# Retention output turned by its own matmuls, the mean of the layer norm spread by a matmul, and the inverse deviation moved behind the second MLP layer

## What is computed

```python
# retention: q, k, v are (2, 8, 768, 64)
for t in range(S):
    state = gamma * state + outer(k[:, :, t], v[:, :, t])
    y[:, :, t] = scale * q[:, :, t] @ state
x = y.transpose(0, 2, 1, 3).reshape(2, 768, 512)
# layer norm and MLP: 512 -> 2048 -> 512
mu = mean(x); var = mean((x - mu) ** 2)
xn = (x - mu) / sqrt(var + 1e-06) * g_ln
x = x + maximum(xn @ w_ch1, 0) @ w_ch2
# then the mixture of four causal attention experts, x (2, 768, 512) -> (2, 768, 512)
```

## Time and profile before

| what | value |
|---|---|
| median of 3 executions | 479.29 us (479.22 to 479.84) |
| the profiled execution | 479.44 us, its span 477.7 us, mean granted TensorE clock 0.998 |
| PE busy | 465.1 us (97%), 2850 matmul records |
| DVE busy | 257.0 us (54%), 595 instructions |
| ACT busy | 148.2 us (31%) |
| POOL busy | 133.1 us (28%) |
| DMA | 33.06 MB moved |

### The profile page before, as it was taken

One profiled execution on the slowest core, in us unless ns is written; L12 is line 12 of the kernel. 1 busy time (PEld: TensorE's weight loads), 2 busy tenths in 40 slices (PEclk: granted clock), 3 DMA queues, 4 the chain that ended last, 5 costly groups with the idle time before them and its releaser, 6 DMA issues.

```text
span 477.7 us, 7612 instructions
## 1 busy us (share of the span) xinstructions
PE 465.1 (97%) x2850; PEld 404.1 (85%) x2850; DVE 257.0 (54%) x595; ACT 148.2 (31%) x338; POOL 133.1 (28%) x165
## 2 busy tenths in 40 slices
PE   7999999999999999999999999999999899999896
PEld 6899988888888888888888888888999799998775
DVE  4657763222556536524673441142637889888833
ACT  2323323111111311111121111131425777777833
POOL 1000009999920000000002000000501567666710
PEclk9999999999999999999999999999999999999999
DMA  7968403444400000000013000000145444443024
GB/s 170 259 150 191 125 1 97 138 130 134 123 0 1 0 0 0 0 0 0 0 33 78 1 0 1 0 1 0 23 100 123 117 116 109 101 103 76 1 105 161
DMA packets 65793, 33.06 MB, mean 69 GB/s; under 512 B 47584, under 2 KB 61920, under 8 KB 65760
## 3 DMA queue, kind: packets, MB, share of 16 engines
q1 hardware_dynamic: 64960, 32.43, 26.6%
q10 hardware_dynamic: 800, 0.20, 0.2%
HBM read 20.03 MB, written 3.15 MB: 49 GB/s over the span
## 4 chain that ended last, share of the span: by engine, by line
PE 88%; DVE 6%; ACT 2%; issue 2%; POOL 1%; DMA 0%; POOLq 0%; ACTq 0%; DVEq 0%
PE ps L708 27%; PE ps L717 27%; PE ps L784 5%; PE ps L631 5%; PE ps L835 4%; PE ps L756 3%; PE ps L803 3%; PE ps L605 3%; PE ps L818 2%; PE ps L592 2%; PE ps L862 2%; DVE a L1448 2%; PE ps L622 2%; PE ps L645 1%; DVE a_low_lo L1456 1%
## 5 line engine op out<-in xcount | busy, mean ns | idle before, releaser
L1302 DVE SCALAR_TENSOR_TENSOR h_t_lo<-ps,h_t_hi 128x512 fp32r<-128x512 f32 x48 | 33.2, 692 | 146.5 <-ACT h_t_hi L992 146.5
L992 ACT ACTIVATE h_t_hi<-ps 128x512 fp32r<-128x512 f32 x48 | 28.7, 598 | 218.3 <-PE ps L708 218.3
L708 PE MATMUL ps<-xn_t_hi,w_hi 128*128 128x512 f32 x192 | 74.8, 389 | 0.0
L708 PE MATMUL ps<-xn_t_hi,w_lo 128*128 128x512 f32 x192 | 74.7, 389 | 0.0
L708 PE MATMUL ps<-xn_t_lo,w_hi 128*128 128x512 f32 x192 | 74.7, 389 | 0.0
L717 PE MATMUL ps<-w_hi,h_t_hi 128*128 128x512 f32 x192 | 74.7, 389 | 0.0
L717 PE MATMUL ps<-w_lo,h_t_hi 128*128 128x512 f32 x192 | 74.7, 389 | 0.0
L717 PE MATMUL ps<-w_hi,h_t_lo 128*128 128x512 f32 x192 | 74.7, 389 | 0.0
L550 POOL TENSOR_SCALAR a<-a,inv_den,weight 128x768 f32<-128x768 f32 (+5 forms) x48 | 34.1, 720 | 50.5 <-DVE inv_den L1468 50.1
L717 PEld LDWEIGHTS ps<-w_hi,h_t_hi 128*128 128x128 f32 x192 | 36.0, 188 | 7.5
L717 PEld LDWEIGHTS ps<-w_lo,h_t_hi 128*128 128x128 f32 x192 | 36.1, 188 | 7.5
(11 more groups left out here) (143 smaller groups left out, 879.0 us busy)
## 6 DMA issues: line engine op xcount, KB each, us to landing
raw_w<-in_moe_w_ch SPq DMA_DIRECT2D x32, 256.0 KB, 3.0
k_twice_hi<-pj_hi SPq DMA_DIRECT2D x32, 96.0 KB, 2.1
k_twice_lo<-pj_lo SPq DMA_DIRECT2D x32, 96.0 KB, 2.2
out_y<-out_sb SPq DMA_DIRECT2D x12, 256.0 KB, 2.0
raw_k<-in_k SPq DMA_DIRECT2D x7, 384.0 KB, 4.6
raw_q<-in_q SPq DMA_DIRECT2D x7, 384.0 KB, 5.1
raw_v<-in_v SPq DMA_DIRECT2D x7, 384.0 KB, 3.4
q_both<-pj_hi SPq DMA_DIRECT2D x16, 96.0 KB, 2.0
```

The source lines that it names most:

```text
L708: mm = pe.matmul(ps[:, f % 2, :], w1[a_][:, f, kk, :], xn_t[b_][:, kk, :], start=(kk == 0 and p_ == 0), stop=(kk == KT - 1 and p_ == 2))
L992: act.activation(h_t["hi"][:, f % 2, :], ps[:, f % 2, :], ACT.Relu).then_inc(s_hhi, 1)
L1302: dve.scalar_tensor_tensor(h_t["lo"][:, f % 2, :], ps[:, f % 2, :], 0.0, f32(h_t["hi"][:, f % 2, :]), ALU.max, ALU.subtract).then_inc(s_hl ...
```

## The change

- **Retention output turned.** In `chunk_outputs`, `raw["v"]` becomes the stationary operand (64 columns) and `prob` the moving one (128 columns), so the result has head dimensions as rows and positions as columns. The two heads of a pair go to the two halves of the PSUM partitions. In `state_outputs` the state is stationary and `q_t` moves. The two heads' states are laid as two blocks of a 128x128 matrix with zeros elsewhere, so one matmul serves both heads: 40 matmuls in place of 80. `chunk_outputs` now stands ahead of `state_outputs`.
- **States.** DVE writes each state in two halves (partitions 0 to 63 and columns 0 to 63, then 64 to 127 and 64 to 127): 2 copies and 8 additions a pair, where there were 1 and 4. POOL clears `state` and fills `mean_of` with 1/512 at the start.
- **Mean by matmul.** `x` now holds the turned output. DVE adds the four pairs of heads of a batch (`first_sum`; `add_heads` later), PE multiplies the sum by `mean_of`, which gives the mean on every partition (`first_mean` twice for block 0, 256 columns each; `next_mean` in blocks 0 and 1, 512 columns), DVE subtracts it (`centred`), and the split into high and low parts reads `centred`.
- **Inverse deviation behind the second layer.** Since relu(a*z) = a*relu(z) for a > 0, the factor `rstd` is applied to the block's result: the residual step becomes `rows = ps * rstd + rows`. `rows` is `x` turned back by DVE (`turn_rows`, 16 squares in slices f = 5 to 7 of the same block). Moments, root and Newton step move to slices 8 to 11 of the same block. Block 2, which had none of it, now has it too.
- **Removed:** `turn_first` (16 PE transposes), `turn_xn` (16 DVE transposes for each of blocks 1 and 2), the whole norm of block 0 ahead of the MLP. `turn_x2` takes slices 2 to 4 in place of 2 to 7.
- POOL's weight splitting now waits for the last `first_sum` in place of `xn`.

The diff, cut to its core:

```diff
             def chunk_outputs(it, g):
                 wait_loaded(pe, it, "v", g)
                 pe.wait_ge(s_prob, 2 * it + g + 1)
+                if it >= 1:
+                    pe.wait_ge(s_yx, y_turn(it - 1, g) + 1)
                 for c in range(G):
                     for j in range(2):
-                        mm = pe.matmul(y_bank(it, g, j)[:, c], prob[:, g, j, c, :], raw["v"][:, it % RB, j, G * g + c],
-                                       start=False, stop=True, skip_group_check=True)
+                        rows_ = slice(j * D, (j + 1) * D)
+                        pe.matmul(y_bank(g)[rows_, c * P:(c + 1) * P], raw["v"][:, it % RB, j, G * g + c], prob[:, g, j, c, :],
+                                  start=(c == 0), stop=(g == 0 and c == 0), skip_group_check=True)
+            def state_outputs(it, g):
+                pe.wait_ge(s_st, 2 * (NC - 1) * (it + 1))
+                for c in range(max(1, G * g), G * g + G):
+                    mm = pe.matmul(y_bank(g)[:, (c - G * g) * P:(c - G * g + 1) * P], state[:, it % 2, c - 1, :],
+                                   q_t[:, it % 2, c, :], start=False, stop=True, skip_group_check=True)
                 mm.then_inc(s_y, 1)
+            def first_mean(b):
+                pe.wait_ge(s_const, 6)
+                pe.wait_ge(s_acc, (HP - 1) * (b + 1))
+                pe.matmul(half_of(mean_bank(), b), mean_of[:, :], half_of(head_sum, b), start=True, stop=True,
+                          skip_group_check=True).then_inc(s_mean, 1)
...
-            key_values(0)
             for it in range(NIT - 1):
                 scores_of(it, 1)
-                state_outputs(it, 0)
+                if it == 0:
+                    key_values(0)
                 chunk_outputs(it, 0)
                 if it == NIT - 2:
                     key_values(it + 1)
+                state_outputs(it, 0)
                 for unit in range(0 if it == 0 else 2, 4):
                     turn(it + 1, unit)
                 scores_of(it + 1, 0)
+                chunk_outputs(it, 1)
                 if it < NIT - 2:
+                    key_values(it + 1)
                     state_outputs(it, 1)
-                    chunk_outputs(it, 1)
-                    key_values(it + 1)
                     for unit in (0, 1):
                         turn(it + 2, unit)
+                if it == HP:
+                    first_mean(0)
...
             def mlp(i, last):
                 for f in range(2, NF):
                     hidden(i, f)
                     project(i, f - 1)
+                    if not last and f == 12:
+                        next_mean(i)
...
# DVE
                 for c in range(1, NC - 1):
-                    dve.wait_ge(s_st, (NC - 1) * it + c)
-                    dve.tensor_tensor(state[:, it % 2, c], kv_bank()[:, c], state[:, it % 2, c - 1],
-                                      ALU.add).then_inc(s_st, 1)
+                    for j in range(2):
+                        half = slice(j * D, (j + 1) * D)
+                        dve.wait_ge(s_st, 2 * (NC - 1) * it + 2 * c + j - 1)
+                        dve.tensor_tensor(state[half, it % 2, c, half], kv_bank()[half, c], state[half, it % 2, c - 1, half],
+                                          ALU.add).then_inc(s_st, 1)
...
+                b, kk = divmod(it - 1, HP)
+                if it >= 2 and kk > 0:
+                    first_sum(b, kk)
+                if it == HP + 1:
+                    for kk in range(KT):
+                        first_centre(0, kk)
+                if it == HP + 2:
+                    for kk in range(KT):
+                        first_lo(0, kk)
                 apply_causal(it + 1, 0)
...
                 for tau in range(NT):
                     dve.wait_ge(s_o, NT * i + tau + 1)
-                    dve.tensor_tensor(xn_tile(tau), ps[:, 2 + tau, :].rearrange("p (k d) -> p k d", k=KT),
-                                      tile_of(i, tau), ALU.add).then_inc(s_x2, 1)
+                    dve.scalar_tensor_tensor(rows_tile(tau), ps[:, 2 + tau, :].rearrange("p (k d) -> p k d", k=KT),
+                                             rstd[:, tau:tau + 1], rows_tile(tau), ALU.mult, ALU.add).then_inc(s_x2, 1)
```

More of the change, by code:

```diff
@@ L118, in retention_moe_program @@
         g_col = sb(ctx, "g_col", [P, KT])
-        with ExitStack() as early:
-            state = sb(early, "state", [P, 2, NC - 1, D])
         with ExitStack() as late:
@@ L607, in scores_of @@
                 mm.then_inc(s_s, 1)
-            def state_outputs(it, g):
-                pe.wait_ge(s_st, (NC - 1) * (it + 1))
-                if y_first(it, g) == 0:
-                    pe.wait_ge(s_turned, 4 * NIT)
-                elif (it, g) == (NIT - 1, 1):
-                    pe.wait_ge(s_yx, y_turn(NIT - 1, 0) + 1)
-                elif y_turn(it, g) >= 1:
-                    pe.wait_ge(s_yx, y_turn(it, g))
-                first = max(1, G * g)
-                for c in range(first, G * g + G):
-                    for j in range(2):
-                        rows = slice(j * D, (j + 1) * D)
-                        pe.matmul(y_bank(it, g, j)[:, c - G * g], q_t[rows, it % 2, c, :], state[rows, it % 2, c - 1, :],
-                                  start=(c == first), stop=False, skip_group_check=True)
             def chunk_outputs(it, g):
@@ L720, in project, with next_mean @@
                         mm.then_inc(s_o, 1)
+            def next_mean(i):
+                pe.wait_ge(s_acc, (KT - 1) * i + sums_before(2))
+                pe.matmul(mean_bank(), mean_of[:, :], head_sum[:, :], start=True, stop=True).then_inc(s_mean, 1)
             def mlp(i, last):
@@ L1003, in mlp @@
                     hidden_hi(i, f)
-                    if f == 7 and not last:
-                        root(i + 1, 0)
+                    if f == 10:
+                        root(i)
                     if last and f == 12:
@@ L1284, in turn_xn, with moments, inverse @@
-            def turn_xn(n, q_):
+                chain = Chain(dve, s_ln, NORM_STEPS * n)
+                def moments():
+                    dve.wait_ge(s_rows, NQ * (n + 1))
+                    for tau in range(NT):
+                        chain.counted(dve.bn_stats(stats[:, tau, 0, :], rows_tile(tau)))
+                    chain.wait()
+                    for tau in range(NT):
+                        chain.counted(dve.bn_aggr(mean_var[:, tau, :], stats[:, tau, 0, :]))
+                def inverse():
+                    chain.wait()
+                    chain.then(dve.tensor_scalar(veps[:, :], mean_var[:, :, 1], LN_EPS, None, ALU.add))
+                    dve.reciprocal(rvar[:, :], veps[:, :]).then_inc(s_rvar, 1)
@@ L1342, in mlp @@
                     hidden_lo(i + 1, 1)
-            norm = normalise(0)[0]
-            moments, inverse, refine = (norm[n] for n in (slice(0, U), U, slice(U + 2, None)))
             for it in range(NIT - 1):
```

298 lines of the change are left out of this document (130 added, 168 removed).

## The result

The changed kernel takes 483.13 us (median of 4 executions, 482.30 to 483.65) against 479.37 for the kernel before beside it: 1.0075 times the time before, interval 1.0058 to 1.0093. It is slower by 0.75%. The forecast was 474.5, faster by 1%, with a range that ended at 479.0. The profiled execution took 483.22 us, its span is 481.5 us.

A forecast was written before the change was run, and what follows sets the result against it. PE bound the kernel before; after the change a loop of waits through DVE would decide the pairs. 1.15 - 6.15 + 0.2 - 1.5 + 1.5 = -4.8 us from 479.44, median 474.5 us, range 467.5 to 479.0.

The forecast's parts named there:

- the wait in the passage: PE ahead of chunk_outputs(7,0), released by DVE's mask: an idle time of 3.5 us, the new stall of this change.
- the start: Up to scores(1,0), with scores(0,1) ahead of the key values: scores(1,0) at about 16.6, 1.15 us more.
- the loop: Retention's pairs: a circle of waits through DVE takes 6.67 us a pair instead of 7.90, 6.15 us less over five.
- What bounds PE: Retention's steady part: PE is busy for all of a pair's 7.90 us; its sum falls by 1.30 to 6.60.
- the chunk outputs: PE in a retention pair: 0.77 us each, instead of 1.48 and 1.39, with two heads on separate array halves.
- the state outputs: PE in a retention pair: half as many whole-array instructions, 0.74 us for group 1 and 0.49 for group 0.
- The rival of unpaired heads: The two heads' chunk outputs don't run side by side: 1.54 us, PE's pair 8.14, total 484; chance 0.10.
- States: DVE in a retention pair: ten half-state instructions at 0.234 us each, 2.34 us instead of 1.17 for five.
- The rival of overlapping halves: DVE overlaps half states, 0.14 us each, 1.4 a pair; PE's 6.60 decides, total 471.3; chance 0.23.
- The passage: From scores(6,0) to the first `hidden`: 17.9 us instead of 19.39, 1.5 less, with PE's 3.5 us wait inside.
- the clock's fall: Behind the 3.5 us stall, 4.3 us of PE work takes twice that at the lower clock: 478.8; chance 0.10.
- The means: MLP blocks 0 and 1: one `next_mean` of 512 columns each on PE, 0.74 us apiece, 1.5 us more.

## Why half states are dear

Two copies of the kernel before, in which nothing but the five state instructions is cut in two: by partitions as in the change, or by columns. Count, elements and waits are the same in both. No chunk or state output is turned here. The first new instruction below is the cut by partitions (`half` is 64 partitions), the second the cut by columns (`half` is 32 columns); each copy has one of them.

```diff
                 for c in range(1, NC - 1):
-                    dve.wait_ge(s_st, (NC - 1) * it + c)
-                    dve.tensor_tensor(state[:, it % 2, c], ...)
+                    for j in range(2):
+                        dve.wait_ge(s_st, 2 * (NC - 1) * it + 2 * c + j - 1)
+                        dve.tensor_tensor(state[half, it % 2, c], ...)
+                        dve.tensor_tensor(state[:, it % 2, c, half], ...)
```

> The kernel before, with one edit: each state instruction is cut in two by partitions (0 to 63, 64 to 127; 64 columns each), ten a pair in place of five, and each waits only for the one before last, as in the changed kernel. PE's order is as before, so a pair has 2.6 us of idle DVE to take it. The changed kernel's ten took 2.54 us a pair where a wait for the one before last would have let two overlap. Theory: an instruction on the other half of the partitions does not begin until the one ahead has ended, so ten take 2.3 to 2.6 us a pair, against 1.17 now. Rival (it was the zero-padded 128-column layout or the busy PSUM that was slow): ten take 1.4 to 1.7. The pair stays 7.9 us by both, since the states are not on PE's path by more than 0.7 us; total within 1 us of before.

> The kernel before, with one edit: each state instruction is cut in two by columns (0 to 31, 32 to 63, all 128 partitions), ten a pair, each waiting for the one before last: the same count, the same elements and the same waits as the cut by partitions. Theory (the hold comes from the change of partitions): here neighbours overlap, ten take 1.3 to 1.7 us a pair. Rival (each small instruction costs its 0.23 to 0.25 whatever it touches): 2.3 to 2.6 us, as by partitions. Total within 1 us of before by both.

The timeline of DVE, by partitions first, then by columns:

```profile
62.85 0.48 DVE L1168 COPY state<-ps 64x64 f32<-64x64 f32 x2 [1.33 <-PE ps L645]
63.36 2.00 DVE L1173 TENSOR_TENSOR state<-ps,state 64x64 f32<-64x64 f32 x8
65.39 0.56 DVE L288 TENSOR_TENSOR scaled_k<-raw_k,decay_sb 128x384 f32<-128x384 f32 x1
```

```profile
50.80 0.29 DVE L1168 COPY state<-ps 128x32 f32<-128x32 f32 x2 [1.34 <-PE ps L645]
51.03 0.97 DVE L1173 TENSOR_TENSOR state<-ps,state 128x32 f32<-128x32 f32 x8
51.91 0.56 DVE L288 TENSOR_TENSOR scaled_k<-raw_k,decay_sb 128x384 f32<-128x384 f32 x1
```

From the copy to the scaling, ten take 65.39 - 62.85 = 2.54 us by partitions and 51.91 - 50.80 = 1.11 us by columns, 0.25 and 0.11 each. The half with 64 columns is longer than that with 32 by 32 x 1.04 ns = 0.03 us, which leaves 0.11 of the 0.14. So the price is in the change of partitions from one instruction to the next, not in the number of instructions. Nor is an addition on half the partitions slow in itself: its record lasts 0.222 us, that of a whole one 0.224. By columns, ten cost no more than the five whole ones of the earlier trace rows (1.17). The Trainium skill, VectorE: DVE Perf Modes, section "Two Vector instructions with no wait between them", states such a hold for an instruction that starts in another quadrant of partitions than the one before. The two traces agree with it, 0.25 us against 0.11. The theory holds, and "small instructions cost a fixed price" falls.

On the total I was wrong by partitions: 497.05 us (one execution), not within 1 us. The states of the kernel before are on PE's path after all: its state outputs wait for them, as they do not in the earlier trace rows.

```profile
56.31 0.66 PE L622 MATMUL ps<-state,q_t 64*128 64x64 f32 x8 [0.93 <-DVE state L1173]
```

The scores start at 49.93 and 59.04, so a pair takes 9.11 in place of 7.90 even where the clock is at 1.00, and the table of stretches shows it far below that in others:

```profile
16.00:24.00 8.00, 7.97 (x79) 6.76 (x79) 2.80 (x8) 3.22 (x8) 0.00 (x0) 0.75 0.82 186
40.00:48.00 8.00, 8.00 (x66) 7.25 (x64) 3.46 (x13) 1.47 (x3) 0.00 (x0) 0.54 0.52 118
```

By columns the time is 479.32 us (one execution), that of before (479.49).

## Start and passage: one edit each

Three versions of the changed kernel with its half states. First, `key_values(0)` stands ahead of `scores_of(0, 1)` again:

```diff
+            key_values(0)
             for it in range(NIT - 1):
                 scores_of(it, 1)
-                if it == 0:
-                    key_values(0)
```

> Changed kernel, but key_values(0) stands ahead of scores_of(0,1) again, as before the change. Theory 1: states(0) begin 0.9 us earlier, so scores(1,0) comes about 0.9 us earlier, 482.2 us. If the start's loss is the lower clock that follows PE's waits of 2.0 and 0.7 us there, the shorter waits may keep the clock up, and then it is 2 to 2.5 us earlier: 480.7 us.

Measured: 481.23 us median of 10 (479.20 to 483.30), 1.0033 of before (1.0013 to 1.0052). In the profiled execution scores(1,0) start at 16.47, 1.48 sooner: 0.94 because the key values run at 9.42 and not at 10.36, as the theory has it, the rest because the clock stayed up. But the wait in the passage is there as before, and this time the clock did not fall behind it (table of stretches, and PE's timeline):

```profile
64.00:66.00 2.00, 0.83 (x13) 0.69 (x13) 1.36 (x3) 0.00 (x0) 0.00 (x0) 1.00 0.00 0
66.00:68.00 2.00, 2.00 (x24) 1.88 (x22) 0.43 (x1) 0.98 (x2) 0.24 (x1) 1.00 0.03 8
```

```profile
65.17 0.88 PE L622 MATMUL ps<-prob,raw_v 128*64 128x128 f32 x12 [2.96 <-issue]
65.97 1.38 PE L631 MATMUL ps<-q_t,state 128*128 128x128 f32 x10
```

Same wait, 2.96 against 2.97 us; chunk outputs 0.88 against 1.55. The ten executions go with their mean granted clock: 479.2 and 479.5 us at 0.999; 480.4 to 481.0 at 0.995; 481.5 to 483.3 at 0.988 to 0.992. So behind two waits of one length the clock fell in one profile and not in the other, and one kernel differs from itself by 4 us.

Second, the splits of batch 0 move behind the mask of (7,0):

```diff
-                if it == HP + 2:
-                    for kk in range(KT):
-                        first_lo(0, kk)
                 apply_causal(it + 1, 0)
+                if it == HP + 2:
+                    for kk in range(KT):
+                        first_lo(0, kk)
```

> Changed kernel, but DVE's four splits of batch 0 (first_lo) stand behind the mask of (7,0) in place of ahead of it. Theory 1 (PE's wait of 3.0 us ahead of chunk_outputs(7,0) is DVE's queue): the wait falls by 1.65 us to 1.3 and the total by 1.6 us if the clock falls all the same, and by about 3.2 us (to 480) if the shorter wait keeps the clock at full. Rival (the wait has another cause, such as the states of pair 7): no change.

Measured: 480.11 us (479.00 to 480.77), 1.0008 (0.9998 to 1.0017), no difference from before. The wait is 1.37 in place of 2.97 and the clock is at 1.00 behind it, both as expected; the fall at the start is still there (0.50 at 18 to 20 us).

```profile
66.09 0.88 PE L622 MATMUL ps<-prob,raw_v 128*64 128x128 f32 x12 [1.37 <-issue]
66.89 1.38 PE L631 MATMUL ps<-q_t,state 128*128 128x128 f32 x10
```

Third, PE is kept busy in that wait with 22 transposes of the identity:

```diff
+            pe.wait_ge(s_turned, 4 * NIT)
+            for _ in range(22):
+                pe.transpose(ps[:, 0, 0:P], ident[:, :], ident[:, :])
             chunk_outputs(NIT - 1, 0)
```

> Changed kernel, and PE turns the identity 22 times into a free bank in its 3.0 us wait ahead of chunk_outputs(7,0); nothing else changes. If the granted clock of 0.50 behind that wait costs what the rows say (chunk outputs of 1.55 in place of 0.81 us, state outputs of 2.15 in place of 1.4), the clock stays at full and the total falls by 1.4 to 1.6 us, to 481.6. If the clock does not matter there because DVE ends last in the passage, no change.

Measured: 482.17 us (481.96 to 482.47), 1.0053 (1.0036 to 1.0069). Behind the fillers the ten state outputs take 1.38 in place of 2.23, yet the time is only 1.0 lower. Passage and MLP together gained 1.9 us between the profiles; the start lost 0.8 (0.4 of it lies ahead of scores(0,1) already, the rest is a fall of the clock that lasted longer than in the changed kernel), the last stage 0.3. The last run therefore fills all of PE's long waits: sixteen transposes ahead of the first state outputs, four ahead of the next turn, and the 22.

```diff
+                if it == 0:
+                    for _ in range(16):
+                        pe.transpose(ps[:, 7, 0:P], ident[:, :], ident[:, :])
                 state_outputs(it, 0)
                 for unit in range(0 if it == 0 else 2, 4):
+                    if it == 0:
+                        for _ in range((4, 0, 0, 0)[unit]):
+                            pe.transpose(ps[:, 7, 0:P], ident[:, :], ident[:, :])
                     turn(it + 1, unit)
```

> The changed kernel as it is, with idle transposes of the identity in PE's waits and nothing else: sixteen ahead of the first state outputs and four ahead of the first turn that follows, and 22 in the wait ahead of chunk_outputs(7,0) (these alone gave 482.17, with the clock falling at the start). Theory: without either fall of the granted clock the start gives back 1.4 and the passage 1.5: 483.1 - 2.9 = 480.2, between 479.8 and 480.8; scores(1,0) begins at 16.6 to 17.0. The rest of the loss against the forecast is then DVE's: pairs of 7.07. Rival (the clock is no cause of its own, the fillers only lengthen the path): 482 to 483.

Measured: 480.44 us median of 10 (479.89 to 480.69), 1.0017 (1.0007 to 1.0027). All ten executions have a clock of 0.998 or more and lie within 0.8 us of each other. So keeping the clock up, with what moved behind it, was worth 2.7 of the changed kernel's 3.8 us, and the rival, that fillers only lengthen the path, falls. Scores(1,0) began at 17.82, though, not at 16.6 to 17.0. Part of that is where the work begins: scores(0,1), ahead of all fillers, start at 9.90 against 9.49. From there to scores(1,0) it takes 7.92 us in place of 8.46, and the pair behind 7.49 in place of 8.20, together 1.25 of the 1.4 expected. Passage and MLP together take 1.86 less, where 1.5 was expected; the first split of batch 1 takes 0.48 there and not 1.48, so not all of it is the clock.

## POOL beside DVE

POOL's weight splitting waits for the fifth head sum in place of the sixth.

```diff
-            pool.wait_ge(s_acc, sums_before(1))
+            pool.wait_ge(s_acc, 5)
```

> The changed kernel, with one edit: POOL's weight splitting waits for the fifth of the six head sums in place of the last, so that its first four instructions run some 4 us earlier, beside PE work and a nearly idle DVE, and not beside the splits of batch 1. Theory: the first split of batch 1 (L1238), 1.48 us in the changed kernel, takes 0.47 again, and PE's first product of the MLP that waits for it comes 0.7 to 1.0 us sooner: 482.3 against 483.1. Rival (the split is slow for a reason of its own): it stays at 1.2 to 1.5 us and the time at 483.1, or the load of w_lo still sets the start.

Measured: 482.62 us (481.99 to 483.51), 1.0067 (1.0050 to 1.0084); the interval does not tell it from the changed kernel. The timeline says why:

```profile
69.72 1.27 POOL L494 TENSOR_TENSOR w_lo<-raw_w,w_hi 128x512 fp32r<-128x512 f32 x1
70.02 1.25 DVE L1226 TENSOR_TENSOR head_sum<-head_sum,x 128x256 f32<-128x256 f32 x1 [3.03 <-ACT x L939]
74.24 0.48 DVE L1238 SCALAR_TENSOR_TENSOR xn_t_lo<-centred,g_col,xn_t_hi 128x256 fp32r<-128x256 f32 x1 [0.25 <-ACT xn_t_hi L951]
```

The split of batch 1 is back at 0.48, as the theory has it, but now the last head sum, 0.42 elsewhere, takes 1.25 beside POOL, and `first_mean(1)` waits for it. The contention is real and it only moved.

## All edits together, and a faster kernel

Whole states, key values first, splits late, POOL at the fifth sum (all as above):

> The changed kernel with four edits together: whole states (64 columns, five DVE instructions, state outputs as two matmuls on the array's quarters), key values ahead of the second scores in the first pair, batch 0's splits behind the mask of (7,0), and the weight splitting at the fifth head sum. Whole states alone gave 475.15. Theory, from its rows: the start 0.5 to 0.9 us sooner, the 1.12 us wait ahead of chunk_outputs(7,0) gone (1.0), the second split of batch 1 at 0.47 in place of 1.17 (0.5 to 0.7): 473.0, between 472.5 and 474. Rival: pairs are bound by PE at 6.93 us and the passage by the chain mask, chunk outputs, sum, mean, centring, so that the earlier edits are absorbed: 474.5 to 475.2.

Measured: 473.30 us (472.86 to 475.09), 0.9868 of before (0.9851 to 0.9884). The theory's 473.0 was right; the profiled execution is the one of 475.09, in which the clock fell at the start (pair 1 took 8.32 in place of 6.93). POOL still meets DVE twice. The next run differs only in `pool.wait_ge(s_acc, 3)`:

> As the kernel with all edits together (473.3), but POOL's weight splitting waits for the third head sum only, so that its first four instructions run at 51 to 57 us, where DVE has slack, as soon as the weights have landed. Theory: the two-input additions of POOL and of DVE hold each other up wherever they meet, so moved to the pairs, they cost PE nothing; the sum ahead of the second mean takes 0.42 in place of 0.77 and the first split of batch 1 0.48 in place of 1.25, and the MLP begins 0.9 us sooner: 472.4. Rival: the scalings that they now meet are stretched instead, and a pair is late by 0.4 to 0.8: 473 to 473.5.

Measured: 473.11 us (472.62 to 474.06), 0.9873 (0.9857 to 0.9890). That is not the theory's 472.4, and the medians don't tell the two kernels apart; the rows do. From scores(7,0) to the first `hidden` it takes 65.74 - 57.99 = 7.75 us against 68.16 - 59.82 = 8.34. The scalings that POOL now meets are stretched, at no cost to PE, whose pair takes 57.99 - 50.49 = 7.50 us there against 59.82 - 52.31 = 7.51 in the run above (timeline of POOL and DVE):

```profile
53.89 0.61 POOL L492 TENSOR_SCALAR w_hi<-raw_w 128x512 fp32r<-128x512 f32 x1
54.03 0.87 DVE L289 TENSOR_TENSOR scaled_k<-raw_k,decay_sb 128x384 f32<-128x384 f32 x1
54.58 1.46 POOL L494 TENSOR_TENSOR w_lo<-raw_w,w_hi 128x512 fp32r<-128x512 f32 x1
54.83 1.63 DVE L289 TENSOR_TENSOR scaled_q<-raw_q,decay_sb 128x384 f32<-128x384 f32 x1
```

The ends fit a turn-taking of whole instructions (a scaling alone takes 0.55): POOL's first ends at 54.50 and DVE's at 54.90, 0.40 later; POOL's second, 1.46 and not 1.27, at 56.04, DVE's second at 56.46, 0.42 later. The Trainium skill has this in SBUF — State Buffer, section "SBUF: two separate sides": a DVE instruction with two SBUF inputs and a GpSimd one that reads SBUF lock each other out for a whole instruction. The rows agree, and masks and centrings, which read PSUM, were not stretched. My expectation was of 0.9 us and 0.6 came.

The same kernel with eleven transposes of the identity in the first pair:

```diff
                 for unit in range(0 if it == 0 else 2, 4):
+                    if it == 0:
+                        for _ in range((4, 7, 0, 0)[unit]):
+                            pe.transpose(ps[:, 7, 0:P], ident[:, :], ident[:, :])
                     turn(it + 1, unit)
```

> As the run with the weight splitting at the third head sum, with eleven idle transposes of the identity (0.12 us each) added to PE's waits in the first pair, four ahead of the first turn and seven ahead of the second. Theory: the granted clock fell to the lower level at 15 to 18 us because PE had stood idle at 12 to 14; kept busy, it stays at the upper level, scores(1,0) takes 0.94 in place of 1.65 and its chunk outputs 0.88 in place of 1.55, 1.4 us less than without them: 471.0. Rival: the clock falls or not whatever PE does in those 2 us (it stayed up in the run with whole states alone, with the same idle time): same as without them, or 0.3 more for the added transposes.

Measured: 472.78 us (472.58 to 472.92), 0.9859 (0.9843 to 0.9876), the lowest median of this study, 6.7 us below before, though not told apart from the run above (lowest times 472.58 and 472.62). The 471.0 of the theory was too low: without fillers the clock did not fall in the profiled execution either (1.00 in all of 8 to 22 us), so there was nothing to win in the median, as the rival had it. Scores(1,0) came 0.27 later, but scores(0,1), ahead of all fillers, were 0.26 later already (10.00 against 9.74), so the fillers lengthened nothing. The four executions lie within 0.34 us of each other, against 1.44 and 2.23 in the two runs above. In the run with 2.23 the clock is behind that (0.996 in the slowest, 0.999 or 1.000 in the others); in the one with 1.44 it is not (0.998 to 1.000 in all four), so what the fillers did for evenness stays open.

## The price of the mean

```diff
+                pe.matmul(mean_bank(), mean_of[:, :], head_sum[:, :], start=True, stop=True)
                 pe.matmul(mean_bank(), mean_of[:, :], head_sum[:, :], start=True, stop=True).then_inc(s_mean, 1)
```

> As the run with the weight splitting at the third head sum, with next_mean issued twice in each of the two blocks (the same product into the same place). It prices that matmul by its own difference. Four passes: 2 x 0.91 = 1.82 us more than without. My forecast's value: 2 x 0.74 = 1.48 more. If it were hidden: nothing.

Measured: 474.42 us (474.38 to 474.79). Against the run without the second product the medians differ by 1.31, the lowest times by 1.76, and the spans of the two profiled executions by 472.7 - 470.9 = 1.8 us. The medians are blurred by the 1.44 us between the four executions without it. The rows are finer: from one mean to the next it takes 221.84 - 133.88 = 87.96 us without the second product and 222.75 - 133.97 = 88.78 with it, so the added one costs 0.82, while the first costs 0.92 here as in the changed kernel. Both lie above my 0.74. The Trainium skill counts four passes in FP8 and Floating Point Precision, section "TensorE Precision Notes". By that count the estimate is 4 x 0.227 = 0.91; the first product agrees, the repeated one comes a little cheaper.

## The prediction, step by step

Three steps failed: the wait in the passage was priced by its length, with the clock behind it at nothing in the sum; the start was given too short a chain and no thought of the clock; and the small terms of the loop were each taken from rows in which the step ran without waiting.

- **What bounds PE, the chunk outputs, the state outputs: right.** Chunk outputs take 0.71 to 0.81 from start to start (forecast 0.77); the state outputs of group 1 take 36.25 - 35.48 = 0.77 (0.74), those of group 0 0.55 (0.49). The rival of unpaired heads fell.
- **States: right in kind, small by 0.20 a pair.** The rival of overlapping halves fell. I took 0.234 from the whole instruction; held ones take 0.254.
- **The loop: right in form, 7.07 for 6.67.** The 0.40 are states +0.20; scalings and mask +0.13 (2.02 for 1.89: the mask starts 0.12 behind the second scaling); from the mask to PE +0.09 (0.14 for 0.05); scores +0.10 (0.87); chunk outputs -0.06; key values with the copy -0.06. Each is a few hundredths taken from a row where the step ran without waiting. A circle that decides has no slack, so all of them count, five times: 2.0 us. The first pair adds the rest: 8.20 behind a fallen clock, 7.49 with PE kept busy.
- **The start: step failed, +2.52 for +1.15.** Of the 1.35 by which scores(1,0) came later than worked out, 0.40 lie ahead of the states (11.28, forecast 10.88), 0.19 in the states (2.53), and 0.76 between the first scaling and the scores: 3.27 us for 2.51, where it takes 2.73 with PE kept busy. So 0.54 are the clock and 0.22 a chain through turns and ACT's copies that I made too short. Of the first 0.40, 0.23 are that scores(0,1) began at 9.49 and not 9.26; in five versions of the changed kernel that do not differ up to there it is 9.06 to 9.93, so this need not be an effect of the change. The start had also the other long wait of PE (2.02 us), which I did not name: I had said that DVE hides PE there, and did not ask what the clock does.
- **The passage: step failed, +1.65 for -1.5.** The wait was there, released by DVE's mask, 2.97 for 3.5. What failed is what follows it: I had taken the clock's fall as a rival at 0.10 and gave it 4.3 us at once. In the profile it is there, and at the start too; all four executions of the changed kernel have the same mean clock, 0.992. The rival's 478.8 was also counted wrongly: it is within 1 us of before, so its 0.10 does not fit the 0.05 for "within". And the range took each rival alone, while here the fall came on top of terms that were too small. From chunk_outputs(7,0) to the scores of (7,1) it takes 71.06 - 67.42 = 3.64 us with the fall and 68.65 - 66.53 = 2.12 with PE kept busy: 1.5 of the 3.1 missed here; 0.4 is that the wait ended later than worked out (12.9 after scores(6,0), not 12.5). Some 1.0 is POOL, an estimate from the split's 1.48 for 0.47: I wrote that it starts 3 us ahead of `hidden`, as now, and did not ask what DVE runs beside it. Before, these were splits that read PSUM; now they read SBUF twice. Where POOL was moved away, in the kernel with whole states, 0.6 came back.
- **The means: term mis-sized**, 0.92 for 0.74 each, 0.36 us in all. The rest of the MLP is as forecast: PE does not wait in it (87.04 busy of 87.04 us above), and DVE's new work is hidden.
- **The last stage: not foreseen, +0.73, and open.** It shows as an issue of SP's queue of 1.95 us where most of its kind take 1.24, and a wait of PE ahead of a product that reads `k_twice` (timeline of SP's queue and of PE):

```profile
356.86 1.24 SPq L428 DMA_DIRECT2D k_twice_hi<-pj_hi  x2
358.79 1.95 SPq L433 DMA_DIRECT2D k_twice_lo<-pj_lo  x2
362.37 0.47 PE L803 MATMUL ps<-k_twice_hi,q_both 128*128 128x512 f32 x1 [0.80 <-issue]
```

Such a wait of PE, of 0.8 to 1.2 us ahead of L803's product, is in the profile of each version of the changed kernel with half states, in none with whole states, and in neither the kernel before nor its two copies; the last stage takes 0.7 to 1.0 us longer where it is. The kernel before has a long issue too, behind which PE does not wait:

```profile
360.03 2.12 SPq L431 DMA_DIRECT2D k_twice_lo<-pj_lo  x2
```

and with whole states there is one of 1.86 us. So a long issue alone does not explain the wait. What makes it long, and why it falls there with half states, was not tried.

In sum, of the 8.6 us between forecast and result some 3.0 are in the pairs and 1.4 in the start, 3.1 in the passage, 0.4 in the MLP and 0.7 in the last stage. Across them, the clock is 2.7 us by the run that keeps PE busy (with what moved behind it), about 2.0 the loop's small terms, and up to 1 POOL beside DVE; the last stage, the means and the small terms of the start, of the first pair and of the passage are the rest. Without the falls the change would still not have won: 480.44 against 479.46. With whole states it wins 4.5 us (475.15 against 479.61), and PE decides again, at 6.93 us a pair (forecast for PE alone 6.60).

## What to carry to other kernels

Split an engine's work by columns, not by partitions, when consecutive small DVE instructions alternate; and when a change turns PE's full occupation into a loop through another engine, size every link of that loop from the end it releases, since each hundredth counts once a turn. Look at each new wait of PE twice: once for its length, once for the clock behind it, which cost 1.5 us behind the wait of 2.97 here and differs from execution to execution. When one part of a large change is suspected, take it out alone: whole states turned a loss of 3.8 us into a gain of 4.5. Moving a POOL instruction moves its contention, so put it where the DVE instruction that it meets has slack.

## What was not expected of the hardware

- Two waits of PE of the same length (2.97 and 2.96 us), in front of the same work: behind one the granted clock was 0.50 for 2 us, behind the other 1.00. With PE's long waits filled, ten of ten executions stayed at 0.998 or above.
- Ten DVE instructions of 128x32 that wait for the one before last start 0.11 us apart; of 64x64 on alternating halves, 0.25 us apart.
- Five kernels that do not differ up to there begin scores(0,1) at 9.06 to 9.93 us in their profiles: 0.9 apart, as much as some of the edits were worth.
- A POOL instruction with a single SBUF input (L492, 0.61 us) holds up a DVE addition just as one with two does, and DVE holds up POOL (1.46 for 1.27).
